# Value and state products in 32-channel tiles at x's partitions, and an order of their own for the first two periods

## The reference

```
f = sigmoid(f_logit)
for t in range(S):
    state = f[t][:, None] * state + outer(k[t], v[t])      # per batch and head, 48 x 48
    y[t]  = q[t] @ state
x = y, heads side by side: (3072, 384)
h = x @ w_in;   x = where(h > 0, h, exp(min(h, 0)) - 1) @ w_out
h = x @ w2_in;  out = (max(h, 0) ** 2) @ w2_out
```

## Time and profile before

| | |
|---|---|
| median of 3 runs | 1005.52 us (1005.23 to 1006.14) |
| profiled execution, its own time | 1007.56 us |
| its span, first to last instruction | 1005.6 us |
| PE busy | 962.6 us (96%), 11076 matmul records |
| DVE, ACT, POOL busy | 538.2, 391.9, 295.7 us |
| mean granted TensorE clock | 0.983 |

### The profile page before, as it was taken

The page is one execution under the profiler, slowest core; times in us unless marked ns, Lnnn a source line. Parts: engine busy times, 40 slices in busy tenths (PEclk is TensorE's granted clock), DMA queues, the critical chain, the costliest instruction groups (busy, mean ns, idle before and its releaser), DMA issues.

```text
span 1005.6 us, 25907 instructions
## 1 busy us (share of the span) xinstructions
PE 962.6 (96%) x11076; PEld 824.0 (82%) x11076; DVE 538.2 (54%) x763; ACT 391.9 (39%) x704; POOL 295.7 (29%) x240
## 2 busy tenths in 40 slices
PE   5758979999999999999999999999999999999998
PEld 4656868888888888888787878999999999999997
DVE  6666787867777686766425663333333333333332
ACT  2424445534443453444444443232242332422322
POOL 4446474635344363535323542000000000000000
PEclk9959999999999999999999999999999999999999
DMA  7241343130222123020003332000010010010000
GB/s 248 90 123 49 103 124 108 43 99 24 79 76 58 55 78 101 23 59 33 18 13 125 99 86 72 1 32 32 1 63 0 16 47 0 31 31 0 32 1 31
DMA packets 47236, 57.95 MB, mean 58 GB/s; under 512 B 7968, under 2 KB 39456, under 8 KB 47136
## 3 DMA queue, kind: packets, MB, share of 16 engines
q1 hardware_dynamic: 44448, 45.63, 15.1%
q10 hardware_dynamic: 2688, 10.85, 3.0%
HBM read 42.30 MB, written 9.44 MB: 51 GB/s over the span
## 4 chain that ended last, share of the span: by engine, by line
PE 87%; DVE 6%; issue 3%; ACT 2%; DMA 1%; POOL 0%; SPq 0%; DVEq 0%; ACTq 0%; POOLq 0%
PE ps L1288 8%; PE ps L1287 8%; PE ps L1292 8%; PE ps L1326 7%; PE ps L1325 7%; PE ps L1329 7%; PE ps L866 6%; PE ps L991 5%; PE ps L1012 5%; PE ps L993 5%; PE ps L998 5%; PE ps L1014 5%; PE ps L1018 5%; PE ps L917 1%; PE ps L882 1%
## 5 line engine op out<-in xcount | busy, mean ns | idle before, releaser
L1241 DVE TENSOR_TENSOR g<-g 128x512 f32<-128x512 f32 x96 | 67.1, 699 | 264.0 <-ACT g L1161 264.0
L576 POOL TENSOR_TENSOR glo<-g,ghi 128x512 fp32r<-128x512 f32 x80 | 109.4, 1367 | 236.0 <-ACT ghi L436 236.0
L1161 ACT ACTIVATE g<-ps 128x512 f32<-128x512 f32 x112 | 67.1, 599 | 284.7 <-PE ps L1292 280.4
L1287 PE MATMUL ps<-xhi,wts 128*128 128x512 f32 x336 | 131.9, 393 | 0.7 <-ACT xhi L421 0.7
L1288 PE MATMUL ps<-xhi,wts 128*128 128x512 f32 x336 | 131.9, 393 | 0.0
L1326 PE MATMUL ps<-wts,ghi 128*128 128x384 f32 x380 | 128.9, 339 | 0.0
L1325 PE MATMUL ps<-wts,ghi 128*128 128x384 f32 x380 | 127.6, 336 | 0.0
L866 PEld LDWEIGHTS ps<-q,k 48*62 48x62 f32 (+6 forms) x4992 | 83.1, 146 | 47.1 <-issue 41.3
L866 PE MATMUL ps<-q,k 48*62 48x32 f32 (+6 forms) x4992 | 90.1, 229 | 29.7 <-issue 17.1
L429 ACT ACTIVATE e<-ps 128x512 f32<-128x512 f32 x80 | 47.8, 598 | 138.7 <-PE ps L998 138.5
L991 PE MATMUL ps<-xhi,wts 128*128 128x512 f32 x240 | 99.3, 414 | 0.6 <-POOL wts L569 0.6
(11 more groups left out here) (109 smaller groups left out, 1651.5 us busy)
## 6 DMA issues: line engine op xcount, KB each, us to landing
raw<-w SPq DMA_DIRECT2D x64, 192.0 KB, 2.4
q<-qk SPq DMA_DIRECT2D x24, 256.0 KB, 4.6
gate<-fl SPq DMA_DIRECT2D x11, 512.0 KB, 4.0
k<-qk SPq DMA_DIRECT2D x11, 512.0 KB, 3.7
v<-vn SPq DMA_DIRECT2D x12, 384.0 KB, 4.4
x<-xo ACTq DMA_DIRECT2D x6, 768.0 KB, 3.3
xs<-x ACTq DMA_DIRECT2D x6, 768.0 KB, 4.3
out<-PT SPq DMA_DIRECT2D x24, 192.0 KB, 1.9
```

Of the source, the lines that this page charges most:

```text
L576: nc.gpsimd.tensor_tensor(out=glo[:, f % 2, :], in0=g[:, f % 2, :], in1=ghi[:, f % 2, :].bitcast(F32), op=ALU.subtract).then_inc(s_glo, 1)
L1287: nc.tensor.matmul(h, w(0, k), xhi[:, k, :], start=(k == 0), stop=False)
```

## The change

**y in place.** Channels are cut into 12 blocks of 32. Block m*4+g lies at partitions 32g to 32g+31 of x's channel group m, and the products now write y there, in PSUM. A block may straddle two heads; then two products add into it, each with the other head's columns zero. For that `vz` holds the values with zeros beside each pair of heads, loaded by 8 DMAs a unit (`load_padded_v`); `state` holds each head's columns at their own channel place and zeros in the other head's rows, 384 wide instead of 192. `q_state` becomes two parts of 16 matmuls around `new_state`, `values` 96 matmuls instead of 48 (without the wait on `s_half`), `last_column` 24 instead of 16 over all 128 partitions, into y's own PSUM banks. `y_copy` is one ACT copy from PSUM straight to `xs`; `last_copy`, `ys`, `v_first`, `gather` and its DMAs are gone. `state_update` is two DVE instructions instead of one, `decay_state` is twice as wide. The level products run the two halves of a unit's token range in another order, in equal number.

**Chunk 0.** x's split reads PSUM directly (`first_x_split`, 4 ACT and 4 DVE instructions). The first loads are in another order, and SP waits for levels of unit (0,1) before it issues the later ones.

**The first two periods** have their own order on every engine. `hidden(1,0)` stands after level 0 of unit (1,0); levels 1, 2, 3 stand between feed-forward blocks, each behind one hidden block; the three groups stand two slots apart instead of three. The gates of units (2,0) and (2,1) are sigmoids on ACT (with table loads) instead of exp, add and reciprocals.

```diff
         def values(c, h):
...
+            for step in range(3):
+                z, at = (step, HP * step) if step < 2 else (0, HP)
+                for i in range(4):
+                    for group in range(4):
+                        m, a, j, third = list(shares(group))[i]
+                        for u in range(UB):
+                            rows = slice(HP * (1 - u), HP * (2 - u))
+                            scores = PT[rows, h % 2, j, 2 * a + z, :] if step < 2 else cross(c, h)[rows, j, a * HP:(a + 1) * HP]
+                            last = nc.tensor.matmul(
+                                banks[32 * group:32 * group + 32, u, m * CELL + at:m * CELL + at + HP],
+                                vz[rows, h % 2, z, a, 32 * (third + j):32 * (third + j) + 32], scores,
+                                start=(fresh and step == 0 and i == 0), stop=(step == 2 and i == 3), skip_group_check=True)
...
+        def q_state(c, h, part):
+            if part == 0:
+                pe.wait_ge(*level(s_q, c, h, LEVELS - 1))
+                pe.wait_ge(s_state, count(c, h, 1, -1))
+                pe.wait_ge(s_krow, count(c, h, 1, 1))
+            else:
+                pe.wait_ge(s_u, count(c, h, 1, 1))
...
+        def y_and_state(c, h):
+            q_state(c, h, 0)
+            new_state(c, h)
+            q_state(c, h, 1)
+            values(c, h)
...
         def period(c, h):
...
             feed(c, h, (9, 10))
-            q_state(c, h)
-            new_state(c, h)
-            values(c, h)
-            feed(c, h, (11,))
+            y_and_state(c, h)
+            feed(c, h, (11, 12))
             last_column(c, h)
-            feed(c, h, (12, 13, 14, 15))
+            feed(c, h, (13, 14, 15))
+
+        def first_period():
+            feed(1, 0, (1, 3))
+            product(1, 0, 1)
+            feed(1, 0, (4, 5))
+            product(1, 0, 2)
+            feed(1, 0, (6, 7))
+            product(1, 0, 3)
+            feed(1, 0, (8, 9))
+            group(1, 0, 0)
+            feed(1, 0, (10, 11))
+            group(1, 0, 1)
...
+        def first_x_split():
+            for b in range(B):
+                act.wait_ge(s_last, b // 2 + 1)
+                nc.scalar.activation(xhi[:, :, b * C:(b + 1) * C], y_cells(ps[:, PAIR_Y + b:PAIR_Y + b + 1, :])[:, 0, :, :],
+                                     ACT.Copy).then_inc(s_xhi1, 1)
...
         def last_column(c, h):
+            pe.wait_ge(s_y, count(c, h, 1, 1))
...
+                for block in range(4 * KD):
+                    m, group = divmod(block, 4)
+                    a = block // 3
+                    last = nc.tensor.matmul(pair(c, h, "Y")[32 * group:32 * group + 32, u, m * CELL + C:(m + 1) * CELL],
+                                            state[:, 2 * (h % 2) + u, 32 * block:32 * block + 32],
+                                            q_last[:, h % 2, u * PAIRS + a:u * PAIRS + a + 1],
+                                            start=False, stop=True, skip_group_check=True)
```

More of the change, by code:

```diff
@@ L293, in load_weights_beside @@
             load_weights(i + 4 for i in split_at(c, f) if i + 4 < 2 * NF)
-        def gather(c, h, heads=range(H)):
-            sp.wait_ge(s_ys, count(c, h, 2, 2))
-            sp.wait_ge(s_lasty, count(c, h, 1, 1))
-            if past(c, h, 2):
-                sp.wait_ge(s_xlo, c * KD)
-            for to, at in moves(c, h, heads):
-                sp.dma_start(to, at).then_inc(s_x, 16)
         def period(c, h):
@@ new lines, in second_period @@
+        def second_period():
+            ffn_step(8)
+            hidden_copies(1, 9)
+            y_copy(1, 0)
+            high(1, 9)
+            split_weights(split_at(1, 9))
+            ffn_step(10)
+            take5(1, 1)
+            hidden_copies(1, 11)
+            gates(1, 3, True)
+            nc.scalar.activation(warm[:, 1:2], warm[:, 0:1], ACT.Exp)
+            high(1, 11)
+            split_weights(split_at(1, 11))
+            take6(1, 1)
+            ffn_step(12)
+            krow_copy(1, 1)
+            ffn_step(13)
+            y_copy(1, 1)
+            ffn_step(14)
@@ L510, in _ @@
         split_weights(range(2))
+        gates(1, 0, True)
+        split_weights(range(2, FIRST_SPLIT))
+        gates(1, 1, True)
+        nc.scalar.activation(warm[:, 1:2], warm[:, 0:1], ACT.Exp)
         take4(0, 0)
         take4(0, 1)
-        gates(1, 0, True)
         take5(0, 0)
@@ L849, in product @@
[L849 to L866 removed]
+            banks, k_all, q_all = level_pair(c, h, l), keys_of(c, h), queries(c, h)
@@ new lines, in product @@
+            for x in range(X if l < 6 else PAIRS):
+                a, z = (x // 2, x % 2) if l < 6 else (x, 0)
+                for n, j in ((0, 0), (1, 1), (1, 0), (0, 1)):
+                    rows, half = slice(HP * j, HP * j + D), HP * n
+                    at = (1 - n) * PAIRS + a
+                    if l < 6:
+                        m = HP - w if l < 5 else 32
+                        there = q_all[rows, at, HP * z:HP * z + HP].rearrange("p (n two w) -> p n two w", two=2, w=w)[:, :, 1, :]
+                        to = banks[half:half + m, j, x * 32:x * 32 + 32].rearrange("p (n w) -> p n w", w=w)
+                    else:
+                        m = HP
+                        there = q_all[rows, at, HP:C]
+                        to = banks[half:half + m, j, a * HP:a * HP + HP]
+                    last = nc.tensor.matmul(to, k_all[rows, at * C + HP * z:at * C + HP * z + m], there,
+                                            start=True, stop=True)
@@ L934, in values @@
-            for u in range(UB):
-                for i in range(2):
-                    for par, j in ((0, 0), (1, 0), (0, 1), (1, 1)):
-                        within(u, i, par, j, par, start=(fresh and u == 0 and i == 0))
-            for u in range(UB):
-                for i in range(2):
-                    for par, j in ((0, 0), (1, 0), (0, 1), (1, 1)):
-                        last = across(u, i, par, j)
-            last.then_inc(s_half, 1)
-            pe.wait_ge(s_half, count(c, h, 1, 1))
@@ L944, in values @@
-            for u in range(UB):
-                for i in range(2):
-                    for par, j in ((0, 0), (1, 0), (0, 1), (1, 1)):
-                        last = within(u, i, par, j, 1 - par, stop=(u == 1 and i == 1))
+            if not past(c, h, 2):
+                pe.wait_ge(*taken(c, h, EARLY))
+            for step in range(3):
+                z, at = (step, HP * step) if step < 2 else (0, HP)
+                for i in range(4):
+                    for group in range(4):
+                        m, a, j, third = list(shares(group))[i]
[6 more added lines that the diff above has]
+                                start=(fresh and step == 0 and i == 0), stop=(step == 2 and i == 3), skip_group_check=True)
@@ L1029, in feed, with group, end_of_levels @@
                     output(c, f - 2)
-        def period(c, h):
-            for i in range(3):
-                product(c, h, 4 + i)
-                if more(c, h):
-                    product(c, h + 1, i)
-                feed(c, h, range(3 * i, 3 * i + 3))
+        def group(c, h, i):
+            product(c, h, 4 + i)
+            if more(c, h):
+                product(c, h + 1, i)
+        def end_of_levels(c, h):
             if more(c, h):
```

602 lines of the change are left out of this document (349 added, 253 removed).

## The result

The changed kernel takes 1039.6 us (median of 4 runs, 1037.7 to 1040.7) against 1005.4 us, a ratio of 1.034, 95% interval 1.032 to 1.036. It is 34 us slower where 11 us faster were forecast, far outside the range of 978 to 1004. The profiled execution has a span of 1038.7 us.

The account below looks back on a forecast made before the run. PE was taken as the bound from 173.55 us on, with all gains before that. Span 1005.6 - 20.2 (start) + 7.7 (first two periods) + 1.2 (ordinary periods) = 994.3, forecast 994 us, range 978 to 1004.

Parts of the forecast that it names:

- Piece 3: Eight ordinary periods after hidden(1,15), PE full: +0.15 us a period, bounds -0.1 to +0.3, +1.2 us for eight.
- values at 8.7 ns: Values in ordinary periods: 192 records at level 5's 8.7 ns each take 1.67 us.
- self-wait: Ordinary periods: the second part of q_state waits for new_state, +0.27 us.
- Piece 1: Kernel start to hidden(1,0): gather and five level products leave the path; start falls from 72.2 to 52.0 us, gaining 20.2.
- 51.4 us for the last column: Chunk 0: y's and state's steps are the same matrix work in bulk and end where they end now.
- upper bound of 54.5: Start of hidden(1,0) if PE's 2.49 us gap comes with more DVE delay; 50.3 if the gap goes.
- Piece 2: First two periods, hidden(1,0) to hidden(1,15): 88.5 us of work plus 20.5 of stalls, 109.0 us, 7.7 more than before.
- the links: First two periods: hidden block to next level's keys, 6.7 us for a single level, 8.5 for a group's second level.
- 88.5 us: PE's pure work in the first two periods: 89.9, less 4.1 for absent output blocks, plus 2.7 for levels 1 to 3.
- A: Rival for the first two periods: links shorten without the reciprocals, 8 us of stalls, start at 51: 980 us; chance 0.20.
- B: Rival: lower clock returns, or hidden(1,0) finds weights or instructions late: start 55, first two periods 114, 1003 us; chance 0.18.
- C: Rival: narrow matmuls in values and q_state cost by count, +2.2 us a unit, 1018 us; chance 0.10.

Follow-up runs that it names:

- experiment 1: Changed kernel with hidden and output blocks put between the parts of y's products in the eight ordinary periods, same instructions: 1029.9 us, ratio 1.023 to the kernel before.
- experiment 4: Changed kernel with GpSimd and VectorE splitting weights behind the level steps in the first two periods: 1027.4 us.
- experiment 6: Kernel before, with GpSimd and VectorE splitting weights behind level and state steps in chunk 1's two periods: 998.4 us, ratio 0.992.
- Experiment 5: Changed kernel with blocks between y's products in every period and chunk 1's weight splits behind level steps: 1011.9 us, ratio 1.006 to the kernel before.
- experiment 8: Changed kernel with five wide products nobody reads added ahead of each of values' three steps, outside chunk 1: 1059.5 us.

## Why the prediction was wrong, point by point

**Piece 3 is the failed step that weighs most.** The prediction summed it from the pace of single products, values at 8.7 ns, q_state unchanged, and a self-wait of 0.27, and got +0.15 us a period with bounds of -0.1 to +0.3. Measured: +3.0. (Its terms add up to 0.12.) Of the 3.0, 2.1 are idle time, 16.5 us in eight periods, and come from a resource the sum had no term for: the number of instructions. 160 records in a row became 288. The other 0.9 is work: 8.7 ns should have been 12.1, a term mis-sized by 0.66 us. The self-wait is there but smaller than the 0.27 forecast: q_state's second part starts 0.28 us after new_state's last product, but before the change the step behind new_state came after 0.14 too, so it adds 0.14. q_state adds 0.04 (1.06 us for 1.02), and 0.18 where a block stands behind it (experiment 1). The prediction compared record counts with time per record, never with what the queue can bring. A hint was in its own rows: the 2.49 us gap with "issue" in the earlier trace rows, where the kernel before packs y's steps of two units together; it ends 1.46 us after a packet on the instruction queue. It was read as a gap "which may or may not come again".

**Piece 1: right path, wrong start.** The gather and five level products did leave the path, and x follows the last column within 2 us. But 51.4 us for the last column was carried over unchanged though the records ahead of it had grown from 288 to 496: it ended at 59.2 instead of 51.9. The upper bound of 54.5 allowed for one supply gap, and there were four; 3 us of work were missing too. Nor does the 52.0 follow from its terms: 51.4 and 1.3 are 52.7. And `hidden(1,0)` was forecast at full clock, but the lower level held from 53.4 to 63.6 us. The start at 61.0 is past the 56 that the prediction named as a sign of being wrong.

**Piece 2: the mechanism was right, the size too small.** Stalls behind the links, GpSimd's key update as what ends them, and the split that stands in the link were all forecast, and experiments 4 and 6 show it. Idle time was 16.7 us where the sum had 20.5, but 4.5 of it are supply gaps, so that the links took some 12. Wrong was the work, 88.5 us. Experiment 5, with 96.8 us busy of 106.4 and 6.6 us at the low clock, says some 93.5 to 94.4, by an estimate from it and from experiment 4: two units' own cost of narrow products, some 2 us, was missing, and 3 us or more that I did not take apart. And the lower clock cost some 11 us more (104.9 us busy for the same records). The sum had nothing for it and the bound two falls of 3.5 us each; it fell five times.

**The rivals.** A did not happen. B's "instructions late" was named but priced as one gap. C's amount for one unit (+2.2) was the nearest to the measured 3.0, by luck, since its cause was wrong: eight 32-column tiles do overlap. Its whole time, 1018 us, is still 22 us short. Had C been judged by count, as an upper bound on any cost that goes with the number of instructions, it would have deserved more than 0.10. The range missed since it took C's chance for the chance of all such costs.

The prediction's note on records of one column also misreads its rows: by the earlier trace rows 32 records of one column take 0.54 us and 32 of 48 columns 0.93, so those of one column do not take as long.

The Trainium skill, "Runtime: NRT & Kernel Launch", section "Instruction fetch mechanics", describes a refill in blocks of 256 instructions that the sequencer fetches itself, and calls its cost "mostly hidden". The block size agrees with the 16,384-byte packets of 128 records here. That it is hidden does not hold for a row of short matmuls: the trace has 15.7 us of gaps above 0.25 us in piece 3 alone, and experiments 1 and 8 show what they are.

## What to carry to other kernels

Count instructions as well as time. A row of 160 records of y's steps had no gap in the ordinary periods here, rows of 224 and more had. So where a long stretch of PE work is products at less than some 30 ns each, look for "issue" gaps 128 records apart, and put wide products in between before making anything else cheaper. A change that swaps data movement for twice as many small products has to pay for them twice, at their pace and at the supply's. And in a chain from one engine to another and back, move everything nobody waits for yet behind the step that somebody waits for: that alone was worth 0.8% of the kernel before.

## What the runs showed of the hardware

- PE's instructions come in packets of 16,384 bytes, 128 products. None of the 92 packets of the changed kernel started less than 3.3 us after the one ahead, and one took 0.9 to 1.4 us itself. After an empty spell PE went on 1.2 to 1.6 us after the packet had landed.
- Gaps in y's steps by records in a row: none for 160, 0.9 us a period for 224, 1.05 for 240, 0.7 for 256, 1.8 for 288. It does not rise evenly; why a period has a gap and its neighbour not, I can only ascribe to where the packet's boundary falls, and did not test it.
- Why the packets keep 3.3 us and more apart though each takes about 1 us, the trace suggests without a test: behind the nine gaps in values in piece 3 of the changed kernel the next packet starts 1.1 to 1.5 us after PE goes on. With 0.9 to 1.3 us for the packet and 1.3 to 1.5 until PE goes on again, that is one packet's whole cycle, as if each were asked for when PE begins on the one before. A gap is then what the 128 records ahead leave of the cycle: 3.73 us between the two ends at 264.47 and 268.20, of which the records took 1.48 and the gap is 2.25.
- Eight 32-column tiles overlap: 64x64 products into 32-column tiles follow at 12.1 ns, the same shape into 48-column tiles at 18.6 (1.79 us for 96, with a self-wait of 0.27), some 16 without the wait. Two thirds of the width take some three quarters of the time.
- A change from wide products to narrow ones and back costs about 0.2 us: 0.11 behind the first wide one, 0.09 ahead of the first narrow one.
- Left open: the gap of 3.91 us behind the added work in chunk 0 of experiment 8.
